# Forming the product of the output weights and the attention weights in fp32r passes of split factors, with the splits placed between the gating operations

## What is computed

```
attn_out = windowed causal attention(q, k, v)          # 8 heads of 64
h = max(x @ w_in, 0); u, v = h[..., :512], h[..., 512:]
v_n = (v - mean) / sqrt(var + 1e-6)
v_s = einsum('ts,bsd->btd', w_spatial, v_n) + b_spatial
x2 = (u * v_s) @ w_out                                  # 512 -> 512
logits = x2 @ w_gate; q, k, v = x2 @ wq[e], x2 @ wk[e], x2 @ wv[e]   # 4 experts of 64
out += top-2 weight of expert e * (causal attention(q, k, v) @ wo[e])
```

## Time and profile before

| | us |
|---|---|
| median of 3 runs (610.01, 610.12, 611.67) | 610.12 |
| the profiled execution, as timed | 609.56 |
| its span in the profile | 607.8 |
| PE busy in the span | 561.7 (92%) |
| DVE, ACT, POOL busy | 368.6, 333.4, 260.4 |
| mean granted TensorE clock | 0.992 of full |

### The profile page before, as it was taken

The page is one execution under the profiler, slowest core; times in us unless marked ns, Lnnn a source line. Parts: engine busy times, 40 slices in busy tenths (PEclk is TensorE's granted clock), DMA queues, the critical chain, the costliest instruction groups (busy, mean ns, idle before and its releaser), DMA issues.

```text
span 607.8 us, 12100 instructions
## 1 busy us (share of the span) xinstructions
PE 561.7 (92%) x4416; PEld 481.7 (79%) x4416; DVE 368.6 (61%) x1243; ACT 333.4 (55%) x975; POOL 260.4 (43%) x445
## 2 busy tenths in 40 slices
PE   3797989998999989999999999999999999999895
PEld 1576978598877779999787778999787678999784
DVE  4996452257778873246778873236777884336773
ACT  2876432145668683334768773234767864324662
POOL 5765313024525752243534653252633664151521
PEclk9998999999999999999999999999999999999997
DMA  8900821000000033020000015020000000000001
GB/s 233 262 2 23 238 70 55 25 1 1 36 28 18 2 87 71 0 79 2 23 24 36 1 43 116 1 79 0 20 27 36 2 1 1 1 1 2 1 36 44
DMA packets 29743, 26.23 MB, mean 43 GB/s; under 512 B 5810, under 2 KB 22194, under 8 KB 29684
## 3 DMA queue, kind: packets, MB, share of 16 engines
q1 hardware_dynamic: 29684, 25.46, 15.0%
HBM read 20.74 MB, written 4.72 MB: 42 GB/s over the span
## 4 chain that ended last, share of the span: by engine, by line
PE 75%; DVE 11%; POOL 5%; issue 4%; ACT 3%; DMA 1%; SPq 1%; DVEq 0%; POOLq 0%; ACTq 0%
PE bank L1095 16%; PE bank L1097 16%; PE bank L1096 16%; PE bank L1126 9%; PE bank L1085 9%; PE bank L1111 3%; POOL p L513 2%; DVE neg L934 2%; PE bank L1275 2%; DVE pt_lo L842 2%; PE bank L1276 2%; ACT q L672 1%; POOL ring L430 1%; DVE q L997 1%; DMA kz<-kT 1%
## 5 line engine op out<-in xcount | busy, mean ns | idle before, releaser
L1095 PE MATMUL bank<-pt_hi,vv 128*64 128x128 f32 (+1 forms) x528 | 107.5, 235 | 13.0 <-issue 8.0
L842 DVE TENSOR_TENSOR pt_lo<-bank,pt_hi 128x512 fp32r<-128x512 f32 (+5 forms) x176 | 84.2, 493 | 41.7 <-ACT pt_hi L582 40.1
L430 POOL TENSOR_SCALAR ring<-ring,r 128x256 f32<-128x256 f32 (+2 forms) x160 | 73.8, 474 | 78.9 <-DVE r L792 78.9
L1097 PE MATMUL bank<-pt_hi,vv 128*64 128x128 f32 (+1 forms) x528 | 101.4, 224 | 0.0
L1096 PE MATMUL bank<-pt_lo,vv 128*64 128x128 f32 (+1 forms) x528 | 101.3, 224 | 0.0
L582 ACT CAST pt_hi<-bank 128x512 fp32r<-128x512 f32 (+5 forms) x176 | 72.8, 432 | 51.5 <-PE bank L1126 49.8
L1095 PEld LDWEIGHTS bank<-pt_hi,vv 128*64 128x64 f32 x528 | 71.9, 136 | 27.1 <-issue 20.2
L557 ACT ACTIVATE ring<-ring,neg 128x256 f32<-128x256 f32 (+2 forms) x160 | 75.1, 473 | 16.6 <-DVE neg L780 16.2
L1085 PE MATMUL bank<-kz,q 128*128 128x512 f32 (+2 forms) x160 | 73.9, 551 | 9.6 <-DMA kz<-kT 9.6
L513 POOL TENSOR_SCALAR p<-p,r,wgt 128x128 f32<-128x128 f32 (+4 forms) x80 | 51.9, 653 | 69.9 <-DVE r L792 65.3
L1096 PEld LDWEIGHTS bank<-pt_lo,vv 128*64 128x64 f32 x528 | 72.1, 137 | 8.6 <-issue 2.9
(11 more groups left out here) (143 smaller groups left out, 1614.9 us busy)
## 6 DMA issues: line engine op xcount, KB each, us to landing
q<-qT SPq DMA_DIRECT2D x16, 256.0 KB, 4.2
kz<-kT SPq DMA_DIRECT2D x32, 128.0 KB, 4.4
v_raw<-v SPq DMA_DIRECT2D x16, 256.0 KB, 3.6
out<-o_sb SPq DMA_DIRECT2D x16, 256.0 KB, 2.0
w_in_raw<-w_in SPq DMA_DIRECT2D x2, 1024.0 KB, 7.1
w_cat_raw<-wcat SPq DMA_DIRECT2D x1, 1544.0 KB, 7.0
w_spatial_raw<-wsT SPq DMA_DIRECT2D x1, 1152.0 KB, 10.5
w_outT_raw<-woT SPq DMA_DIRECT2D x1, 1024.0 KB, 5.3
```

Of the source, the lines that this page charges most:

```text
L430: last = nc.gpsimd.tensor_scalar(p, p, r1[0:r, i % 2, h:h + 1], 0.0, ALU.mult, ALU.add)
L842: last = nc.vector.tensor_tensor(pt_lo[0:r, g % 2, c0:c1], bank[0:r, 2 + g % 2, c0:c1], pt_hi[0:r, g % 2, c0:c1].bitcast(F32), ALU.subtract)
L1095: nc.tensor.matmul(to, hi_l, hi_r, start=first, stop=False)
L1097: return nc.tensor.matmul(to, lo_l, hi_r, start=False, stop=last)
```

## The change

Both factors are split into high and low parts, and `fold()` uses `three()` with them. `CUT` moves from 384 to 512, so that the column ranges are 512 and 260. The splits go by block d of 128 rows, one block after each of the gatings i = 2, 3, 4 and 5: three copies on ACT and three subtractions on DVE (columns 0 to 512 of `wcat`, its other 260 columns, and 512 columns of `w_out`). The high part of the 260 columns is written over columns 0 to 260 of the raw block, and its low part over columns 512 to 772, so ACT's second copy waits for DVE's first subtraction. The high part of the 512 columns lies in `w_c_hi`, where the result goes later; so ACT copies no result before the first four banks are done. In the diff, `w_cat_v_split` is the buffer of the 260 columns' parts.

```diff
-CUT = CK + P
+CUT = CV
 FOLD = [(t, 0, CUT) for t in range(KT)] + [(t, CUT, CW) for t in range(KT)]
+FOLD_SPLIT_AT = (2, 3, 4, 5)
...
+                def high_fold_inputs(d):
+                    act.wait_ge(s_wcat, 16)
+                    nc.scalar.copy(wc_hi[:, d, 0:CUT], wcat_raw[:, d, 0:CUT]).then_inc(s_fsh, 1)
+                    act.wait_ge(s_fsl, 3 * d + 1)
+                    nc.scalar.copy(wcat_v[:, d, 0:CW - CUT], wcat_raw[:, d, CUT:CW]).then_inc(s_fsh, 1)
+                    act.wait_ge(s_woT, 16)
+                    nc.scalar.copy(woT_hi[:, d, :], woT_raw[:, d, :]).then_inc(s_fsh, 1)
+
                 for i in range(8):
                     high_g(i)
+                    if first and i in FOLD_SPLIT_AT:
+                        high_fold_inputs(FOLD_SPLIT_AT.index(i))
                 if first:
                     for j, (t, c0, c1) in enumerate(FOLD):
-                        act.wait_ge(s_fmm, j + 1)
+                        act.wait_ge(s_fmm, max(j + 1, KT))
...
+                def low_fold_inputs(d):
+                    dve.wait_ge(s_fsh, 3 * d + 1)
+                    nc.vector.tensor_tensor(wc_lo[:, d, 0:CUT], wcat_raw[:, d, 0:CUT], wc_hi[:, d, 0:CUT].bitcast(F32),
+                                            ALU.subtract).then_inc(s_fsl, 1)
+                    dve.wait_ge(s_fsh, 3 * d + 2)
+                    nc.vector.tensor_tensor(wcat_v[:, d, CUT:CW], wcat_raw[:, d, CUT:CW],
+                                            wcat_v[:, d, 0:CW - CUT].bitcast(F32), ALU.subtract).then_inc(s_fsl, 1)
+                    dve.wait_ge(s_fsh, 3 * d + 3)
+                    nc.vector.tensor_tensor(woT_lo[:, d, :], woT_raw[:, d, :], woT_hi[:, d, :].bitcast(F32),
+                                            ALU.subtract).then_inc(s_fsl, 1)
+
                 for i in range(8):
...
+                    if first and i in FOLD_SPLIT_AT:
+                        low_fold_inputs(FOLD_SPLIT_AT.index(i))
...
             def fold():
-                pe.wait_ge(s_fold, 32)
                 for j, (t, c0, c1) in enumerate(FOLD):
                     if j == KT:
                         pe.wait_ge(s2_g, 8)
                     for d in range(KT):
-                        last = nc.tensor.matmul(bank[:, FOLD_BANKS[j], 0:c1 - c0], woT_raw[:, d, P * t:P * t + P],
-                                                wcat_raw[:, d, c0:c1], start=(d == 0), stop=(d == KT - 1))
+                        if j == 0:
+                            pe.wait_ge(s_fsl, 3 * (d + 1))
+                        hi = wcat_v[:, d, 0:CW - CUT] if c0 else wc_hi[:, d, 0:CUT]
+                        lo = wcat_v[:, d, CUT:CW] if c0 else wc_lo[:, d, 0:CUT]
+                        last = three(bank[:, FOLD_BANKS[j], 0:c1 - c0], woT_hi[:, d, P * t:P * t + P],
+                                     woT_lo[:, d, P * t:P * t + P], hi, lo, d == 0, d == KT - 1)
                     last.then_inc(s_fmm, 1)
...
                 for i in range(4):
+                    if first and i:
+                        pe.wait_ge(s_flo, KT + 1 + i)
                     qk_product(i)
-                    if first and i == 0:
-                        pe.wait_ge(s_flo, 2 * KT)
```

More of the change, by code:

```diff
@@ L170, in build @@
         wcat_raw = sb("w_cat_raw", [P, KT, CW], F32, at)
+        wcat_v = sb("w_cat_v_split", [P, KT, CW], F32R, at)
         ring = sb("ring", [P, SLOTS1, 2 * P], F32, at)
@@ L179, in build @@
         woT_raw = sb("w_outT_raw", [P, KT, DM], F32, at)
+        woT_lo = sb("w_outT_lo", [P, KT, DM], F32R, at)
+        woT_hi = sb("w_outT_hi", [P, KT, DM], F32R, at + 4 * KT * DM)
         x_hi = sb("x_hi", [P, KT, S], F32R, at)
@@ L228, in build @@
         s_sel = sem("pool_chain")
-        s_fold = sem("fold_weights_in")
+        s_wcat, s_woT = sem("w_cat_in"), sem("w_outT_in")
+        s_fsh, s_fsl = sem("fold_inputs_hi"), sem("fold_inputs_lo")
         s_win = [sem("w_in_u_in"), sem("w_in_v_in")]
@@ L339, in load_fold @@
                 sp.wait_ge(s1_t, NG1)
-                sp.dma_start(wcat_raw[:], wcat.rearrange("(k p) n -> p k n", p=P)).then_inc(s_fold, 16)
+                sp.dma_start(wcat_raw[:], wcat.rearrange("(k p) n -> p k n", p=P)).then_inc(s_wcat, 16)
                 sp.wait_ge(s2_um, 8)
-                sp.dma_start(woT_raw[:], woT.rearrange("(k p) n -> p k n", p=P)).then_inc(s_fold, 16)
+                sp.dma_start(woT_raw[:], woT.rearrange("(k p) n -> p k n", p=P)).then_inc(s_woT, 16)
             def row(b, first, more):
```

## The result

The changed kernel takes 613.76 us (median of 10 runs, 611.48 to 617.5) against 610.07 us before (10 runs, 608.02 to 611.67). The medians differ by 3.7 us. The ratio of the means is 1.0071, with an interval of 1.0048 to 1.0094: 4.3 us slower, between 2.9 and 5.7.

A forecast was written before the change was run, and what follows sets the result against it. PE was taken to bound the kernel, busy 92% of the span and setting the fold's end. Late splits +1.4 and the clock's fall +1.5 gave +2.9 us on 610.12, thus 613.0 us, range 611.0 to 614.8.

The forecast's parts named there:

- A block takes 3.94 us: Splits on ACT and DVE: each block's serial chain takes 3.94 us, where PE delivers a group every 1.85.
- PE waits twice, and the lateness costs +1.4: Fold: PE waits for blocks 2 and 3, so the matmul behind the fold starts at 124.1 instead of 122.73.
- The matmuls cost 0.235 and 0.118 us, 16.9 in all: Fold on PE: 48 fp32r matmuls of 512 columns and 48 of 260 take 16.9 us, replacing 20.4 us.
- POOL holds up the first subtraction, 0.26 us a block: Splits: POOL's `g_lo` delays DVE's first subtraction; without this each of four blocks is 0.26 us shorter.
- the price without POOL: Rival that POOL does not hold DVE up: lateness +0.4 us, with the clock 1.9, 612.0 us; chance 0.10.
- The clock falls, +1.5: PE's thin stretch before the last block drops the clock to half; 3.5 us under dense work, taken as 1.5 us.
- the prediction's bound of 2.3: Upper end of the clock fall's cost, if the low clock lasts 5 us into the fold's work.
- No cost behind the fold: Behind the fold, the delayed result copies and subtractions cost nothing; everything there moves by the same amount.
- The sum: Whole kernel: +1.4 for lateness and +1.5 for the clock make +2.9 us, forecast 613.0 us.
- that of the clock staying up: Rival: clock stays at 2.4 GHz through the fold, leaving +1.4, 611.5 us; chance 0.17.
- That the splits hide and 3.5 us are won: Rival: splits finish in time and the fold is 3.5 us shorter, 606.6 us; chance 0.03.

The follow-up runs named there:

- the filler kernel: Changed kernel plus 17 throwaway PE matmuls before the fold's waits for blocks 2 and 3; 610.54 us, ratio 1.0002 to the kernel before.
- the interleaved kernel: Changed kernel with splits reordered across groups from gating 0, one PE wait before the fold; 606.43 us with POOL's `g_lo` held back, 607.07 with it in place.
- late `g_lo`: Changed kernel with POOL's `g_lo` of groups 2 and on held until all twelve split subtractions are done; 613.26 us, ratio 1.0047 to the kernel before.
- the profile after: First profiled execution of the changed kernel itself, nothing further changed; span 614.3 us, 33.36 us from gating 2 to the first matmul behind the fold.

## Why the prediction was right

The mechanism was right in each step. The direction, the size (613.0 forecast, 613.76 measured) and the range hold; what follows goes by its own steps, of which one term of the sum was mis-sized.

- *A block takes 3.94 us.* 3.96 measured. The last split was forecast 15.8 us behind gating 2 and came at 112.24 - 96.33 = 15.9.
- *PE waits twice, and the lateness costs +1.4.* 1.41, read from the filler kernel, which has the lateness and not the clock's fall.
- *The matmuls cost 0.235 and 0.118 us, 16.9 in all.* 16.86 in the interleaved kernel, where they run without a wait.
- *POOL holds up the first subtraction, 0.26 us a block.* Right in kind, too large in size: 0.88 against 0.69 is 0.19, and 0.77 us on the fold distance instead of 1.0. The held subtraction itself came as forecast: it ended 98.69 - 98.15 = 0.54 us behind POOL's end, where 0.56 had been taken, and 2.36 us behind the start of the gating, where 2.38 had been. What was off is the same subtraction without POOL, which ends at 2.16 (late `g_lo`) and not at 2.12. So the price without POOL was off, and not the sum. The block of 3.96 is 0.02 longer than forecast: the last two subtractions took 0.43 and 0.69 instead of 0.40 and 0.67.
- *The clock falls, +1.5.* This is the term that was mis-sized. It fell in every profile of the changed kernel, but cost 1.84, 1.89 and 2.47 us, the last a little over the prediction's bound of 2.3. The prediction priced a low stretch of 3.5 us under the work; it was 4.0 us in two profiles and 5.3 in the profile after. The price per us was right: 4.0 x (1 - 0.235 / 0.43) = 1.8.
- *No cost behind the fold.* Right: 485.1 us behind the second cut before, and 484.6, 485.0 and 485.1 in the three profiles of the changed kernel.
- The sum: 1.41 + 1.84 to 2.47 is 3.3 to 3.9 us, where 2.9 was forecast. The medians differ by 3.7, the means by 4.3.

Of the rivals, that of the clock staying up was refuted by the three profiles; the fillers made it true by force, and its price, +1.4, holds. That the splits hide and 3.5 us are won was rightly held impossible in the given order and place. The interleaved kernels show that the gain was real (3.55) and was lost to the order and the late start together; no run separates the two fully.

## What to carry to other kernels

Work that is called hidden between other engines' operations has to be written down as a chain of who waits for whom: here six short instructions of 0.4 to 0.9 us, alternating between two engines, made a group of 3.96 us out of one of 1.85, though DVE was busy for 2.4 us of it and ACT for 1.9. Begin as early as the inputs allow, and let the second engine take up in one group what the first made in the group before: so the same instructions cost nothing here. And where PE has to wait in thin bursts, add to the wait what the clock takes behind it: here that is more (1.8 to 2.5 us) than the lateness itself costs (1.4).

## What the runs showed of the hardware

The clock's fall does not need an unbroken idle stretch: three matmuls (0.7 us) between waits of 1.41 and 2.97 us did not keep it up in any of three profiles, while 17 fillers did. In one of them the clock was already low 0.3 us into the second wait (0.51 from 107.0 to 108.0, and the wait began at 106.7). Nor does the fall have to come in a wait: with `g_lo` late it came 1.3 us after PE had taken up its work again. How much it costs moves from execution to execution at the same instructions. Falls at other places move the time of one execution by nearly as much as this change is worth: the profile after reaches gating 2 3.1 us later than before, with two falls ahead of it. The Trainium skill (TensorE: Matmul & The Clock Gate, Part 1) says that activity releases a clock that is halved by default; the runs agree, in that with the fillers at work in the same stretch the granted clock stayed at 1.00 throughout.

Second, a subtraction on DVE and one on POOL, each with both inputs in SBUF, hold each other up whichever comes first: 0.88 instead of 0.69 us on DVE when POOL was first, 1.33 instead of 0.81 on POOL when DVE was. This agrees with the Trainium skill (SBUF — State Buffer, Who interferes with whom).
